# First attention of a two-layer MLP kernel: where the row sums are finished, when the first weights are loaded, and how long O keeps two banks

## The chip, the cores and the metric

One NeuronCore of a Trainium2 chip runs the whole kernel. The time is device time in microseconds (us) of one execution; the median of three executions is compared. One further execution was recorded by the profiler, and all rows below come from it.

## The reference

```python
scores = cap * np.tanh(scale * np.matmul(q, k.transpose(0, 1, 3, 2)) / cap)     # q, k, v: 2 x 12 x 448 x 64
scores = scores - np.max(scores, axis=-1, keepdims=True)
attn = np.exp(scores)
attn = attn / (np.sum(attn, axis=-1, keepdims=True) + 1e-09)
x = np.matmul(attn, v)                                     # then reshaped to 896 tokens x 768
h = x @ w_in                                               # 768 x 2048
x = np.where(h > 0.0, h, np.exp(np.minimum(h, 0.0)) - 1.0) @ w_out
h = x @ w_in2
return np.maximum(0.01 * h, h) @ w_out2
```

## The kernel before

Everything is float32. A product is made of parts: each operand is split into a high part of type float32r and a low part, which is the rest, and hi*hi, hi*lo and lo*hi are added up.

The attention of the 24 heads and most of the first product of the first MLP run in a common loop of 55 steps s (STEPS), which every engine writes out in its own order. A head h has two halves, k = 2h and 2h + 1; a half is 224 rows of the scores. The work of half k is spread over the steps:

- step k - 1: TensorE (PE) makes the scores of half k (`score`, L1080 and L1081), after the tanh of half k - 1 has left the bank.
- step k: ScalarE (ACT) takes the tanh (L598); VectorE (DVE) takes the maximum of each row (`maxima`, L762).
- step k + 1: ACT takes the exponential, two instructions, with the sums of the rows (`exp`, L608).
- step k + 2: PE transposes the probabilities (`transposes`, L1094); ACT copies the high part out (`p_high`, L617); DVE makes the low part (`p_low`, L769).

The work of a whole head stands at these places:

- step 2h + 3: GpSimd (POOL) adds EPS to the row sums (`denominators`, L544), and DVE inverts them (`invert`, L779). The inverse goes to DRAM by a DMA of 1.8 KB at step 2h + 4 (`store_inv`, L443), and comes back spread over 64 rows at step 2h + 5 (`load_inv`, L460). `invert(h)` waits until the store of head h - 2 has landed, since both use one buffer.
- step 2h + 5: PE multiplies by v (`values`): for h < DIRECT = 8 twelve matmuls with 64 rows of output (L1107 to L1109), else eight with 128 rows (L1112, L1113).
- step 2h + 8, for h < 8: DVE multiplies O by the inverse and stores it (`scale_o`, L787). Step 2h + 6, for h >= 8: DVE adds the two halves of O (`take_o`, L797 and L799). Each ends with the semaphore o_read.
- `x_parts(m)` on POOL splits the rows of two heads, 2m and 2m + 1, at step 4m + 11, or 4m + 9 from m = 4 on. `split_v` on POOL splits v, `split_qk` q and k.

All DMAs but one are issued by SyncE (SP) in one order; an issue that waits holds up all behind it. At step 8 it loads four units of the weights (L466), 384 KB each, and at step 29 three more. Three of them are split early: the high part by DVE at steps 11, 15 and 19 (`w_high`, L809), the low part by POOL at steps 13, 17 and 21.

PSUM has eight banks: two for scores, two for the transposed probabilities, two for O (o_ps), two more (mlp_ps) that serve the odd halves below ALONE_P = 22 and then the MLP. `values(h)` may start when enough heads have been read:

```python
        def o_bank(h):
            return o_ps[:, h % 2 if h < DIRECT else 0, 0:SEQ]

        def o_users(h):

            return h - 1 if h <= DIRECT and h >= 2 else h if h > DIRECT else 0
```

From step 24 on the MLP is mixed in. EARLY names unit and chunks for steps 24 to 30, MIXED for the later ones; a chunk is three matmuls (L1118 to L1120). Units 0, 1 and 2 have the banks mlp_ps 0, mlp_ps 1 and o_ps 1. From about step 24 on PE has work in all gaps, and after the attention come the rest of the MLP and the second one.

Of the kernel before, what the change touches and what calls it, by code (L numbers as in the profile page):

```python
# [9 lines left out]
ALU = mybir.AluOpType  # L10
AX = mybir.AxisListType

BATCH, HEADS, SEQ, HD = 2, 12, 448, 64
# [4 lines left out]
NHEAD = BATCH * HEADS  # L18
# [12 lines left out]
RAW = 4  # L31
RING = 4
AHEAD = 3
# [3 lines left out]
EPS = 1e-9  # L37
# [4 lines left out]
ALONE_P = 22  # L42

DIRECT = 8
EARLY = {24: ((2, (0, 1, 2)),), 25: ((2, (3,)),), 26: ((0, (0, 1, 2)),), 27: ((0, (3,)),), 28: ((1, (0, 1, 2)),),
         29: ((1, (3,)),), 30: ((0, (4,)), (1, (4,)), (2, (4,)))}
STEPS = 55
MLP_BANKS = 3

# [14 lines left out]
def chunks_at(s):  # L64

    if s in EARLY:
        return [], [], EARLY[s]
# [94 lines left out]
def build(nc, qT, kT, v, w, cap, out, inv_rows):  # L162
    with ExitStack() as ctx:
# [15 lines left out]
        row_sum, row_den, row_inv = sb("row_sum", [QT, 2, NQ]), sb("row_den", [QT, 2, NQ]), sb("row_inv", [QT, 2, NQ])  # L179
# [67 lines left out]
        o_ps = pb("o_ps", [P, 2, 512])  # L247
# [12 lines left out]
            return slice((h + 1) % 2 * HD, (h + 1) % 2 * HD + HD)  # L260

        def o_bank(h):
            return o_ps[:, h % 2 if h < DIRECT else 0, 0:SEQ]

        def o_users(h):

            return h - 1 if h <= DIRECT and h >= 2 else h if h > DIRECT else 0

        def bank(i):
            return (scores, probs_t, o_ps, mlp_ps)[i // 2][:, i % 2, 0:SEQ]  # L270
# [13 lines left out]
        def unit_hidden(u):  # L284
# [15 lines left out]
        exp_done, transposed, p_hi_done, p_lo_done = (sem("exp_done"), sem("transposed"), sem("p_hi_done"),  # L300
                                                      sem("p_lo_done"))
        den_done, inv_done = sem("den_done"), sem("inv_done")
# [119 lines left out]
        @block.sync  # L422
        def _(sp):
            def load_k(h):
                if h >= 4:
                    sp.wait_ge(k_split, h - 3)
                elif h >= 2:
                    sp.wait_ge(k0_split, h - 1)
                sp.dma_start(k_raw[:, h % 2, :], kT[h, :, :]).then_inc(k_loaded[h % 2], 16)

            def load_q(h):
                if h >= 2:
                    sp.wait_ge(q_split, h - 1)
                sp.dma_start(q_raw[:, h % 2, :], qT[h, :, :]).then_inc(q_loaded[h % 2], 16)

            def load_v(h):
                if h >= 2:
                    sp.wait_ge(v_split, h - 1)
                sp.dma_start(v_raw[:, h % 2, :], v[h, :, :]).then_inc(v_loaded[h % 2], 16)

            def store_inv(h):
                sp.wait_ge(inv_done, h + 1)
                sp.dma_start(inv_rows[h, :].rearrange("(p t) -> p t", t=NQ), row_inv[:, h % 2, :]  # L443
                             ).then_inc(inv_stored[h % 2], 16)

            def load_inv(h):

                m = h // 2
                sp.wait_ge(inv_stored[h % 2], 16 * m + 16)
                if h < DIRECT:  # L450
                    if h >= 2:
                        sp.wait_ge(o_read, h - 1)
                    rows = inv_all[0:HD, h % 2, :]
                else:
                    if m < DIRECT // 2 + 2:
                        sp.wait_ge(o_read, DIRECT - 1 + m - DIRECT // 2)
                    else:
                        sp.wait_ge(x_scaled, m - 1 - DIRECT // 2)
                    rows = inv_all[hi_rows(h), m % 2, :]
                sp.dma_start(rows, inv_rows[h:h + 1, :].broadcast_to([HD, SEQ])  # L460
                             ).then_inc(inv_loaded[h % 4], 16)

            def load_w(r):
                if r >= RAW:
                    sp.wait_ge(*load_free(r - RAW))
                sp.dma_start(w_raw[:, r % RAW, :], w[RAW_ROWS[r], :, :]).then_inc(w_loaded[r % RAW], 16)  # L466

            load_q(0)
            sp.dma_start(cap_col[:, :], cap.broadcast_to([P, 1])).then_inc(cap_loaded, 16)
            load_k(1)  # L470
            load_q(1)
            load_v(0)
            load_v(1)
            for h in (2, 3):
                load_k(h)
                load_q(h)
            for s in range(STEPS):
                for u in units_ending_at(s - 1):
                    load_w(u + AHEAD + RAW)
                if s % 2 == 0 and s // 2 + 4 < NHEAD:  # L480
                    load_k(s // 2 + 4)
                    load_q(s // 2 + 4)
                if s == 8:
                    for u in range(RAW):
                        load_w(u)
                if s % 2 == 1 and 0 <= (s - 5) // 2 < NHEAD:
                    load_inv((s - 5) // 2)
                if s % 2 == 1 and 2 <= s // 2 + 1 < NHEAD:
                    load_v(s // 2 + 1)
                if s % 2 == 0 and 0 <= (s - 4) // 2 < NHEAD:  # L490
                    store_inv((s - 4) // 2)
                if s == 29:
                    for u in range(RAW, AHEAD + RAW):
                        load_w(u)
            for r in range(units_ending_at(STEPS - 1)[0] + AHEAD + RAW, len(RAW_ROWS)):
                load_w(r)
            for i, (there, rows_half, batch) in enumerate(((y12_done, 0, 1), (y22_done, 1, 1), (y11_done, 0, 0), (y21_done, 1, 0))):
                for t in range(HC):
                    sp.wait_ge(there, HC + t + 1)
                    sp.dma_start(out[rows_half * HC + t, :, batch * SEQ:(batch + 1) * SEQ], y_out[:, HC * i + t, :]  # L500
                                 ).then_inc(y_stored, 16)
            sp.wait_ge(y_stored, 16 * BATCH * KC)

        @block.gpsimd
        def _(pool):
# [23 lines left out]
            def split_v(h):  # L529
                b = h % 2  # L530
                pool.wait_ge(v_loaded[b], 16 * (h // 2) + 16)
                if h >= 2:
                    pool.wait_ge(pv_done, h - 1)
                raw = v_raw[:, b, :].rearrange("p (c d) -> p c d", c=NQ)
                pool.tensor_scalar(v_both[:, b, :, hi_rows(h)], raw, 1.0, 0.0, ALU.mult, ALU.add).then_inc(v_hi_done, 1)
                pool.wait_ge(v_hi_done, h + 1)
                pool.tensor_tensor(v_both[:, b, :, lo_rows(h)], raw, v_both[:, b, :, hi_rows(h)].bitcast(F32), ALU.subtract
                                   ).then_inc(v_split, 1)

            def denominators(h):  # L540
                pool.wait_ge(exp_done, 4 * h + 4)
                if h >= 2:
                    pool.wait_ge(inv_done, h - 1)
                pool.tensor_scalar(row_den[:, h % 2, :], row_sum[:, h % 2, :], EPS, 1.0, ALU.add, ALU.mult  # L544
                                   ).then_inc(den_done, 1)

            def x_parts(m):
                b = m % 2
                pool.wait_ge(o_read, 2 * m + 2)
# [23 lines left out]
            for s in range(STEPS):  # L573
                for u in units_ending_at(s - 1):
                    split_w(u + AHEAD)
                if s % 2 == 1 and 0 <= (s - 3) // 2 < NHEAD:
                    denominators((s - 3) // 2)
                for m in range(PAIRS):
                    if s == x_step(m):
                        x_parts(m)  # L580
                if s % 2 == 0 and s // 2 + 2 < NHEAD:
                    split_qk(s // 2 + 2)
                if s % 2 == 1 and 0 <= s // 2 - 1 < NHEAD:
                    split_v(s // 2 - 1)
                if s in (13, 17, 21):
                    split_w((s - 13) // 4)
            for n in LO_ON_POOL[units_ending_at(STEPS - 1)[0] + AHEAD:]:
# [168 lines left out]
        def _(dve):  # L756
# [16 lines left out]
                    ALU.subtract).then_inc(p_lo_done, 1)  # L773

            def invert(h):
                dve.wait_ge(den_done, h + 1)
                if h >= 2:
                    dve.wait_ge(inv_stored[h % 2], 16 * (h // 2))
                nc.vector.reciprocal(row_inv[:, h % 2, :], row_den[:, h % 2, :]).then_inc(inv_done, 1)  # L779
# [282 lines left out]
        def _(pe):  # L1062
# [59 lines left out]
            def hidden(u, chunks):  # L1122
                pe.wait_ge(*split_done(u))
                if u < 2:
                    pe.wait_ge(p_lo_done, ALONE_P)
                elif u == 2:
                    pe.wait_ge(o_read, DIRECT)
                else:
                    pe.wait_ge(g_done, u - MLP_BANKS + 1)
                for c in chunks:  # L1130
                    x = KC * (u // MAT_UNITS) + c
                    if u % MAT_UNITS < MLP_BANKS:
                        pe.wait_ge(x_lo_done, x + 1)
                    last = product(unit_bank(u), u % RING, c, x_hi[:, x, :], x_lo[:, x, :], c == 0, c == KC - 1)
                if KC - 1 in chunks:
                    last.then_inc(unit_done, 1)
# [125 lines left out]
```

## Time and profile before

| what | value |
|---|---|
| three executions | 584.12, 584.13 and 587.40 us; median 584.13 |
| profiled execution | 588.14 us, its span 586.4 us |
| busy share of the span | PE 96%, DVE 79%, ACT 60%, POOL 48% |
| granted TensorE clock, mean | 0.994 of full speed |

The span is the time from the first to the last instruction. Granted clock 1.00 is 2.4 GHz and 0.50 is 1.2 GHz. PE is shown as busy to the modelled end of each matmul, some 0.37 us after its start, while matmuls of 448 columns follow each other at 0.20 us: an idle time that is shown for PE is about 0.2 us shorter than the delay of the next start.

### The profile page before, as it was taken

To read this page: it belongs to the slowest core of one execution; us is meant where nothing else is said; L and a number is where in the kernel's file an instruction comes from. 1 tells how busy PE (TensorE), PEld (TensorE's weight loads), DVE (VectorE), ACT (ScalarE), POOL (GpSimd) and SP (SyncE) were. 2 spreads that over 40 slices of the span, in tenths; PEclk is the share of its full clock that TensorE was granted. 3 is DMA by queue.
4 is the path that set the end of the run, shared out by engine and by line. 5 is a ranking of instruction groups with operands and counts; after the bars stand their busy time and mean duration, and the time that the engine had idled before them with its cause. 6 is when DMAs were issued, how large, how long until landed. Compare 5 with 4: busy or idle time off the path is not lost. (4 is left out here: it accounts for less than half of the span.)

```text
span 586.4 us, 8605 instructions
## 1 busy us (share of the span) xinstructions
PE 560.9 (96%) x2908; PEld 502.9 (86%) x2908; DVE 463.6 (79%) x707; ACT 354.0 (60%) x606; POOL 283.9 (48%) x297
## 2 busy tenths in 40 slices
PE   7898989999999999999999999989999998999997
PEld 5666769888988999999999999969999997899997
DVE  5788888877776323699898989789999868999881
ACT  6998888889997355655554454355445445554440
POOL 6779998898985676554000000687657530000000
PEclk9999989989999999999999999999999999999999
DMA  6364533545433233333743533022111335446241
GB/s 172 89 186 101 137 95 96 174 123 135 116 82 72 78 107 109 108 107 108 269 135 109 182 90 105 1 88 75 54 55 57 96 91 167 156 135 215 82 157 59
DMA packets 34172, 67.07 MB, mean 114 GB/s; under 512 B 6864, under 2 KB 18768, under 8 KB 34128
## 3 DMA queue, kind: packets, MB, share of 16 engines
q1 hardware_dynamic: 33984, 66.28, 38.0%
q8 instruction: 24, 0.39, 0.3%
q10 hardware_dynamic: 144, 0.23, 0.1%
q14 instruction: 20, 0.16, 0.1%
HBM read 63.70 MB, written 2.80 MB: 113 GB/s over the span
## 5 line engine op out<-in xcount | busy, mean ns | idle before, releaser
L564 POOL TENSOR_TENSOR w_lo<-w_raw,w_hi 128x768 fp32r<-128x768 f32 (+1 forms) x62 | 105.5, 1704 | 52.5 <-ACT w_hi L628 51.9
L564 POOL TENSOR_TENSOR w_lo<-s_sum,w_hi 128x384 fp32r<-128x384 f32 x32 | 37.7, 1191 | 119.1 <-ACT w_hi L628 119.1
L628 ACT ACTIVATE w_hi<-s_sum 128x768 fp32r<-128x768 f32 (+1 forms) x64 | 43.4, 684 | 78.4 <-DVE s_sum L880 52.0
L628 ACT ACTIVATE w_hi<-w_raw 128x768 fp32r<-128x768 f32 (+1 forms) x77 | 56.5, 736 | 31.0 <-PE o_ps L1120 15.7
L608 ACT ACTIVATE soft<-soft,neg_max 112x448 f32<-112x448 f32 x96 | 63.0, 661 | 2.7 <-DVE soft L762 2.7
L762 DVE TENSOR_SCALAR_CACHE_REDUCE soft<-soft,neg_abs 112x448 f32<-112x448 f32 x96 | 60.6, 668 | 2.3 <-ACT soft L598 2.0
L769 DVE TENSOR_TENSOR p_lo<-probs_t,p_hi 112x896 fp32r<-112x896 f32 x37 | 40.3, 1089 | 21.9 <-ACT p_hi L617 21.7
L1118 PE MATMUL mlp_ps<-x_hi,w_hi 128*128 128x448 f32 x132 | 49.7, 376 | 0.0
L1120 PE MATMUL mlp_ps<-x_hi,w_lo 128*128 128x448 f32 x132 | 48.7, 369 | 0.0
L1119 PE MATMUL mlp_ps<-x_lo,w_hi 128*128 128x448 f32 x132 | 48.7, 369 | 0.0
L598 ACT ACTIVATE soft<-scores 112x896 f32<-112x896 f32 x47 | 43.0, 914 | 7.4 <-PE scores L1081 7.4
L1080 PE MATMUL scores<-k_hi,q_stack 128*112 128x448 f32 x94 | 37.3, 396 | 6.2 <-ACT soft L598 6.1
L617 ACT ACTIVATE p_hi<-probs_t 112x896 fp32r<-112x896 f32 x37 | 33.7, 910 | 14.1 <-PE probs_t L1094 14.1
L1094 PEld LDWEIGHTS probs_t<-ident,soft 112*112 112x112 f32 x296 | 30.5, 134 | 11.0 <-issue 6.5
L1094 PE MATMUL probs_t<-ident,soft 112*112 112x112 f32 x296 | 34.8, 261 | 5.1 <-DVE p_lo L769 4.0
L1081 PE MATMUL scores<-k_lo,q_stack 128*112 128x448 f32 x94 | 35.1, 373 | 0.0
L804 DVE SCALAR_TENSOR_TENSOR b<-act_g,mlp_ps 128x448 f32<-128x448 f32 x22 | 13.6, 619 | 27.1 <-ACT act_g L637 27.1
L880 DVE TENSOR_TENSOR s_sum<-w_raw 128x768 f32<-128x768 f32 (+1 forms) x32 | 28.7, 896 | 5.9 <-issue 3.6
L884 DVE TENSOR_TENSOR w_lo<-s_sum,w_hi 128x768 fp32r<-128x768 f32 x32 | 30.5, 953 | 1.3 <-ACT w_hi L628 1.3
L839 DVE TENSOR_TENSOR g_first<-b,g_first 128x896 fp32r<-128x896 f32 x24 | 30.1, 1253 | 0.8 <-ACT g_first L647 0.8
L839 DVE TENSOR_TENSOR g_last<-b,g_last 128x896 fp32r<-128x896 f32 x24 | 27.9, 1163 | 2.2 <-ACT g_last L647 2.2
L635 ACT ACTIVATE act_g<-mlp_ps 128x448 f32<-128x448 f32 x22 | 11.9, 540 | 24.9 <-PE mlp_ps L1120 24.9
(236 smaller groups left out, 1753.1 us busy)
## 6 DMA issues: line engine op xcount, KB each, us to landing
w_raw<-w_units SPq DMA_DIRECT2D x120, 384.0 KB, 3.2
q_raw<-qT SPq DMA_DIRECT2D x24, 224.0 KB, 3.0
k_raw<-kT SPq DMA_DIRECT2D x23, 224.0 KB, 2.7
v_raw<-v_rows SPq DMA_DIRECT2D x24, 112.0 KB, 2.8
inv_all<-inv_rows SPq DMA_DIRECT2D x24, 112.0 KB, 3.1
y_t<-y_out SPq DMA_DIRECT2D x12, 224.0 KB, 2.8
inv_rows<-row_inv SPq DMA_DIRECT2D x24, 1.8 KB, 3.0
k_raw<-kT ACTq DMA_DIRECT2D x1, 224.0 KB, 3.3
```

What stands on the lines that cost most here:

```text
L564: pool.tensor_tensor(w_part(w_lo, n), w_source(n), f32(w_part(w_hi, n)), ALU.subtract).then_inc(w_lo_pool, 1)
L598: nc.scalar.activation(soft[0:QT, k % SOFT, :, :], scores_of(k)[0:QT, :, 0:SEQ], ACT.Tanh, scale=scale_reg).then_inc(tanh_done, 1)
L608: nc.scalar.activation(soft[0:QT, b, t, :], soft[0:QT, b, t, :], ACT.Exp, bias=neg_max[:, c, t:t + 1], scale=-1.0, accum_out=row_sum[:, h ...
L628: nc.scalar.activation(w_part(w_hi, n), w_source(n), ACT.Copy).then_inc(w_hi_done, 1)
L762: nc.vector.tensor_scalar(soft[0:QT, b, t, :], soft[0:QT, b, t, :], neg_abs[0:QT, 0:1], BIG, ALU.mult, ALU.min, accum_out=neg_max[:, c, t: ...
L769: nc.vector.tensor_tensor(p_lo[:, h % 2, :, cols].rearrange("p (a b) q -> p a b q", a=2), probs_of(k)[0:QT, :, 0:SEQ].rearrange("p a (b q) ...
L839: nc.vector.tensor_tensor(parts[:, 2:4, :], g_source(l, n)[0], f32(parts[:, 0:2, :]), ALU.subtract).then_inc(g_split, 1)
L1080: nc.tensor.matmul(dst[0:QT, t, 0:SEQ], q_stack[:, b, rows], k_hi[:, b, :], start=True, stop=False)
L1094: last = nc.tensor.transpose(probs_of(k)[0:QT, c // 2, col:col + QT], soft[0:QT, k % SOFT, t, c * QT:(c + 1) * QT], ident[:, :])
L1118: nc.tensor.matmul(dst, w_hi[:, r, blk], hi, start=start, stop=False)
L1119: nc.tensor.matmul(dst, w_hi[:, r, blk], lo, start=False, stop=False)
L1120: return nc.tensor.matmul(dst, w_lo[:, r, blk], hi, start=False, stop=stop)
```

## The change

The EPS is added on DVE, just ahead of the reciprocal, and not on POOL. The seven first units of weights are loaded one by one at steps 7, 11, 15, 19, 23, 26 and 29. O has two banks for ten heads and not for eight; so units 0 and 1 are begun ahead of unit 2. On POOL `split_v` stands ahead of `x_parts`.

```diff
+TWO_BANKS = 10
-EARLY = {24: ((2, (0, 1, 2)),), 25: ((2, (3,)),), 26: ((0, (0, 1, 2)),), 27: ((0, (3,)),), 28: ((1, (0, 1, 2)),),
-         29: ((1, (3,)),), 30: ((0, (4,)), (1, (4,)), (2, (4,)))}
+EARLY = {24: ((0, (0, 1, 2)),), 25: ((0, (3,)),), 26: ((1, (0, 1, 2)),), 27: ((1, (3,)),), 28: ((2, (0, 1, 2)),),
+         29: ((2, (3,)),), 30: ((0, (4,)), (1, (4,)), (2, (4,)))}
+FIRST_LOADS = (7, 11, 15, 19, 23, 26, 29)
...
         def o_bank(h):
-            return o_ps[:, h % 2 if h < DIRECT else 0, 0:SEQ]
+            return o_ps[:, h % 2 if h < TWO_BANKS else 0, 0:SEQ]
         def o_users(h):
-            return h - 1 if h <= DIRECT and h >= 2 else h if h > DIRECT else 0
+            return h - 1 if h <= TWO_BANKS and h >= 2 else h if h > TWO_BANKS else 0
...
-                if s == 8:
-                    for u in range(RAW):
-                        load_w(u)
...
-                if s == 29:
-                    for u in range(RAW, AHEAD + RAW):
-                        load_w(u)
+                if s in FIRST_LOADS:
+                    load_w(FIRST_LOADS.index(s))
...
-            def denominators(h):
-                pool.wait_ge(exp_done, 4 * h + 4)
-                if h >= 2:
-                    pool.wait_ge(inv_done, h - 1)
-                pool.tensor_scalar(row_den[:, h % 2, :], row_sum[:, h % 2, :], EPS, 1.0, ALU.add, ALU.mult
-                                   ).then_inc(den_done, 1)
...
             for s in range(STEPS):
                 for u in units_ending_at(s - 1):
                     split_w(u + AHEAD)
-                if s % 2 == 1 and 0 <= (s - 3) // 2 < NHEAD:
-                    denominators((s - 3) // 2)
+                if s % 2 == 1 and 0 <= s // 2 - 1 < NHEAD:
+                    split_v(s // 2 - 1)
                 for m in range(PAIRS):
                     if s == x_step(m):
                         x_parts(m)
                 if s % 2 == 0 and s // 2 + 2 < NHEAD:
                     split_qk(s // 2 + 2)
-                if s % 2 == 1 and 0 <= s // 2 - 1 < NHEAD:
-                    split_v(s // 2 - 1)
...
             def invert(h):
+                dve.wait_ge(exp_done, 4 * h + 4)
+                nc.vector.tensor_scalar(row_den[:, h % 2, :], row_sum[:, h % 2, :], EPS, 1.0, ALU.add, ALU.mult
+                                        ).then_inc(den_done, 1)
                 dve.wait_ge(den_done, h + 1)
...
                 if u < 2:
                     pe.wait_ge(p_lo_done, ALONE_P)
                 elif u == 2:
-                    pe.wait_ge(o_read, DIRECT)
+                    pe.wait_ge(o_read, TWO_BANKS)
```

The queue of SP at steps 7 to 9, before: the three rows of head 1 (store, load, v), then k and q of head 8, then the weights, then the store of head 2.

```order
L443 DMA inv_rows<-row_inv 112x4
L460 DMA inv_all<-inv_rows 64x448
L439 DMA v_raw<-v_rows 112x256
L429 DMA k_raw<-kT 128x448
L434 DMA q_raw<-qT 128x448
L466 DMA w_raw<-w_units 128x768 x4
L443 DMA inv_rows<-row_inv 112x4
```

The same place in the changed kernel:

```order
L447 DMA inv_rows<-row_inv 112x4
L464 DMA inv_all<-inv_rows 64x448
L443 DMA v_raw<-v_rows 112x256
L470 DMA w_raw<-w_units 128x768
L433 DMA k_raw<-kT 128x448
L438 DMA q_raw<-qT 128x448
L447 DMA inv_rows<-row_inv 112x4
```

One unit in place of four is ahead of the store of head 2, and it stands ahead of k and q; the next ones stand in the same way ahead of the stores of heads 4, 6, 8 and 10.

PE at step 24, with the semaphores that it waits for (the scores of half 25, then the first chunk of the MLP), before:

```order
L1080 MATMUL scores<-k_hi,q_stack 112x448 [waits tanh_done]
L1081 MATMUL scores<-k_lo,q_stack 112x448
L1080 MATMUL scores<-k_hi,q_stack 112x448
L1081 MATMUL scores<-k_lo,q_stack 112x448
L1118 MATMUL o_ps<-x_hi,w_hi 128x448 [waits x_lo_done,o_read,w_lo_pool]
```

and in the changed kernel:

```order
L1074 MATMUL scores<-k_hi,q_stack 112x448 [waits tanh_done]
L1075 MATMUL scores<-k_lo,q_stack 112x448
L1074 MATMUL scores<-k_hi,q_stack 112x448
L1075 MATMUL scores<-k_lo,q_stack 112x448
L1112 MATMUL mlp_ps<-x_hi,w_hi 128x448 [waits x_lo_done,p_lo_done,w_lo_pool]
```

The first chunk now goes to a bank that the odd halves used, and waits for the low part of half 21 where it waited for the reading of O.

## Rows read from the trace of the kernel before

**Rows 1.** The page's granted TensorE clock, 40 slices of 14.7 us.

```profile
PEclk9999989989999999999999999999999999999999
```

**Rows 2.** Stretches of span: PE, PEld, DVE, ACT, POOL busy us; clock, DMA share, GB/s.

```profile
82.30:85.70 3.40, 3.36 (x10) 2.96 (x11) 3.35 (x10) 1.60 (x5) 3.15 (x6) 0.50 0.60 164
89.00:114.00 25.00, 25.00 (x154) 22.96 (x153) 20.82 (x46) 21.08 (x43) 21.93 (x29) 1.00 0.39 108
...
119.90:123.30 3.40, 3.40 (x11) 3.00 (x10) 3.00 (x6) 3.37 (x6) 3.40 (x3) 0.51 0.87 249
```

**Rows 3.** Timeline, steps 10 to 13: start, length, what, idle before and its releaser.

```profile
38.63 1.09 DVE L769 TENSOR_TENSOR p_lo<-probs_t,p_hi 112x896 fp32r<-112x896 f32 x1 [1.05 <-ACT p_hi L617]
...
39.56 0.43 PE L1080 MATMUL scores<-k_hi,q_stack 128*112 128x448 f32 x1 [0.33 <-ACT soft L598]
...
39.75 0.96 DVE L787 TENSOR_TENSOR x_raw<-o_ps,inv_all 64x448 f32<-64x448 f32 x1
...
40.86 0.39 PE L1107 MATMUL o_ps<-p_hi,v_both 112*64 112x448 f32 x1 [0.27 <-DVE x_raw L787]
...
44.28 0.92 ACT L617 ACTIVATE p_hi<-probs_t 112x896 fp32r<-112x896 f32 x1 [0.66 <-PE probs_t L1094]
...
45.09 0.92 ACT L598 ACTIVATE soft<-scores 112x896 f32<-112x896 f32 x1
```

**Rows 4.** Timeline of PE: first score matmul of steps 9, 13, 15 and 17.

```profile
33.06 0.43 PE L1080 MATMUL scores<-k_hi,q_stack 128*112 128x448 f32 x1 [0.33 <-ACT soft L598]
...
46.16 0.43 PE L1080 MATMUL scores<-k_hi,q_stack 128*112 128x448 f32 x1 [0.33 <-ACT soft L598]
...
53.16 0.43 PE L1080 MATMUL scores<-k_hi,q_stack 128*112 128x448 f32 x1 [0.33 <-ACT soft L598]
...
60.82 0.43 PE L1080 MATMUL scores<-k_hi,q_stack 128*112 128x448 f32 x1 [0.33 <-ACT soft L598]
```

**Rows 5.** Waits of PE, 0 to 190 us: in total, times, longest.

```profile
PE probs_t L1094 <- DVE p_lo L769: 4.0, 4, 1.8
PE o_ps L1107 <- DVE x_raw L787: 2.7, 5, 1.3
```

**Rows 6.** Timeline of SP's queue, steps 6 to 11.

```profile
29.73 0.43 SPq L443 DMA_DIRECT2D inv_rows<-row_inv  x1
32.12 0.45 SPq L460 DMA_DIRECT2D inv_all<-inv_rows  x1
...
35.88 1.86 SPq L466 DMA_DIRECT2D w_raw<-w_units  x4
37.77 0.60 SPq L443 DMA_DIRECT2D inv_rows<-row_inv  x1
43.65 0.45 SPq L460 DMA_DIRECT2D inv_all<-inv_rows  x1
```

**Rows 7.** Timeline of DVE, steps 11 to 14: what waited for a DMA.

```profile
43.73 0.18 DVE L779 RECIPROCAL row_inv<-row_den 112x4 f32<-112x4 f32 x1 [0.69 <-DMA inv_rows<-row_inv]
...
51.03 0.18 DVE L779 RECIPROCAL row_inv<-row_den 112x4 f32<-112x4 f32 x1 [1.11 <-DMA inv_rows<-row_inv]
...
54.43 0.95 DVE L787 TENSOR_TENSOR x_raw<-o_ps,inv_all 64x448 f32<-64x448 f32 x1 [1.04 <-DMA inv_all<-inv_rows]
```

**Rows 8.** Timeline of DVE, PE and ACT, steps 22 to 25.

```profile
78.80 1.09 DVE L769 TENSOR_TENSOR p_lo<-probs_t,p_hi 112x896 fp32r<-112x896 f32 x1 [0.35 <-ACT p_hi L617]
...
79.93 0.96 DVE L787 TENSOR_TENSOR x_raw<-o_ps,inv_all 64x448 f32<-64x448 f32 x1
...
82.34 0.71 PE L1112 MATMUL o_ps<-p_hi,v_both 112*128 112x448 f32 x1 [1.58 <-DVE x_raw L799]
...
83.42 0.67 ACT L608 ACTIVATE soft<-soft,neg_max 112x448 f32<-112x448 f32 x1 [0.94 <-DVE soft L762]
...
88.99 0.93 PE L1094 MATMUL probs_t<-ident,soft 112*112 112x112 f32 x8
```

**Rows 9.** Groups by line, 0 to 190 us: busy us, mean ns, idle before.

```profile
L544 POOL TENSOR_SCALAR row_den<-row_sum 112x4 f32<-112x4 f32 x24 | 4.6, 193 | 2.0
```

## The prediction

> **What bounds the kernel now.** I read the page's clock row first, then the stretches, then the chain of starts in the attention. From 89 to 114 us PE has no idle time at full clock [rows 2]; up to step 24, about 85 us, it waits now and then. So time can only be won ahead of 89 us, and a wait that ends there moves all that follows.
>
> Ahead of step 24 the loop over a head closes like this, read off steps 10 to 13 [rows 3]. The scores start at 39.56, just behind a tanh; `values` of head 3 starts at 40.86, where it would follow the four score matmuls at 40.4 (four at 0.2 and the longer first one). It waits for `scale_o`, which ends at 40.71, and this stands in DVE's order behind `p_low`, which waited 1.05 us for ACT. Everything after `values` is late with it: the transposes, the high part at 44.28 (0.66 us late by ACT's account), and behind it, in ACT's order, the tanh at 45.09, which lets the next scores start. So the distance between two score starts is the price of a head, waits included. With the one at 39.56 [rows 3], the starts 33.06, 46.16, 53.16 and 60.82 [rows 4] give 6.50 (head 2), 6.60 (head 3), 7.00 (head 4) and 7.66 us (head 5). The waits behind them are 2.7 us in five times, the longest 1.3 [rows 5].
>
> Heads 2 and 3 run with no DMA in the way, so 6.50 for an even head and 6.60 for an odd one is what this order costs. Heads 4 and 5 are longer by 0.50 and 1.06. There DVE waited for DMAs: 0.69 and 1.11 us in `invert`, 1.04 in `scale_o` [rows 7]. And there the queue of SP shows why: the store at 29.73 had landed 2.4 us later, when the load that waits for it was issued at 32.12; the store at 37.77, behind four units of weights, landed after 5.9 us, at 43.65 [rows 6]. SP waits at that place, so v, k, q and the next store are late too, which is how head 5 pays.
>
> The second place is step 23. `values(9)` starts at 82.34 after 1.58 us of idle PE, released by the second half of `take_o(8)` [rows 8]: heads 8 and 9 share a bank. The clock is at 0.50 from 82.3 to 85.7, that is 1.2 GHz, and PE is busy for 3.36 of these 3.40 us [rows 2], so this stretch costs 1.7 us. It began when PE took up work after that wait. A like stretch, 119.9 to 123.3, costs 1.7 more [rows 2]; its wait, 1.8 us for `p_low`, is the longest of four [rows 5]. The clock row has these two dips and no other [rows 1].
>
> That bears on the base of the sum. The three times are 584.12, 584.13 and 587.40: the third is 3.3 above the others, about two such stretches (3.4). The profiled execution, 588.14, has both; without them it would be 584.7. I take it that the median, 584.13, has neither.
>
> **The change part by part.**
>
> *Loads one by one.* At step 7 one unit stands ahead of the store of head 2 in place of four. The four made the landing 5.9 instead of 2.4 us, 3.5 for four, so 0.9 us for one: a landing of about 3.3 us. SP reaches that store 1.9 us earlier too, since the one unit now stands ahead of k and q [rows 6]. So it lands at about 35.9 + 3.3 = 39.2. `invert(4)`, which needs it, could start about 43.0 (43.73 less its wait of 0.69 [rows 7]): 3.8 us to spare. The three DMA waits of DVE go, and heads 4 and 5 fall back to 6.50 and 6.60. Gain 0.50 + 1.06 = **1.56 us**, bounds 1.0 (part of head 5's time is POOL's or ACT's) and 2.2 (head 3's wait shrinks also). At step 29 one unit in place of three; PE waits for nothing there (89 to 114 us [rows 2]), so it is worth 0. The units that are split early are wanted at steps 11, 15 and 19, four steps of over 3 us after their load: nothing waits.
>
> *EPS on DVE.* It takes 0.19 us on POOL, 24 times, 4.6 us in all [rows 9]. On DVE the nearest row is the reciprocal of the same tile, 0.18 us [rows 7]. If all of it were seen, it would cost 24 x 0.19 = 4.6 us. But it stands ahead of `maxima` at odd steps, and DVE waits for ACT after that, ahead of `p_low`: 1.05 us at step 10 [rows 3], 0.35 at step 22 [rows 8], where it is tightest. 0.18 fits into 0.35, so I take 0. At step 11 the early `w_high` stands there as well and the margin is nearly used up; 0.1 may show there. The waits of `invert` for POOL go, but DVE waits for ACT next anyway: worth 0 where PE is full.
>
> *Two banks for ten heads.* `values(9)` now waits for `scale_o(7)`, 79.93 + 0.96 [rows 8], so it starts at 81.0, not 82.34: 1.34 us earlier. What is late next? The next point at which PE waits for a vector engine is the transposes of half 23, at 88.99 [rows 8]; 1.7 us of the way there is half clock, so with full clock it stands at 87.3. By PE alone it would now be 86.0. But it needs the low part of half 22: the exponential of half 23 starts at 83.42, held by DVE's `maxima` behind `take_o(8)` (0.94 us [rows 8]), which the bank does not change. Two exponentials and their read-outs take 1.4 us, the high part 0.92, the low part 1.09 [rows 3], the semaphores 0.1: 86.95. So the gain at full clock is 87.3 - 86.95 = **0.35 us**, bounds 0 (EPS on DVE pushes that low part back by 0.18, and more) and 1.34 (if `maxima` gets earlier by itself). In an execution like the profiled one it is 88.99 - 86.95 = 2.05, since the half clock would go with the wait. The first chunk of the MLP, which now waits for the low part of half 21, comes at about 84.3, when DVE has just finished it (it precedes the reciprocal of step 23): at most 0.2 us, inside the margin of the same chain. `values(10)` needs `take_o(8)` only, and `values(11)` as before.
>
> *v first on POOL.* POOL shows no wait that PE pays for in this part; `values` is released by O alone [rows 5]. `x_parts` moves back by about 1.2 us of v and gains 0.3 of the EPS; its rows are first used at step 24, the nearest pair five steps after its split. Worth 0.
>
> Sum: 1.56 + 0.35 = 1.9 us. From the median 584.13 this gives **582.2 us**. For a profiled execution: 588.14 - 1.56 - 2.05 = 584.5 if the second stretch at half clock stays, and 582.8 if both are missing.
>
> **A rule that speaks against the spread loads.** The small store landed after 5.9 us behind four units [rows 6]. The Trainium skill, "DMA: Bandwidth & Descriptors", section "Queues, rings and completion order", says that a completion increment lands only after every earlier write of the same DMA engine; by that rule, the trace agrees, any unit ahead of a store is paid by the store, and now five stores have one ahead of them instead of one store four.
>
> **The rivals.**
>
> *Slower: five stores late instead of one.* Each load ahead of a store delays its landing, and `invert` two heads later waits for it on DVE. If each of the five cost what the worse of the two heads costs, 1.06 us, it would be 5.3 us for a gain of 0.35 at the bank: 584.13 + 5.3 - 1.56 - 0.35 = 587.5. Against it: with a landing of 3.3 us there are 3.8 us to spare. It decides once a store takes longer than about 7.1 us to land.
>
> *Nothing to see.* DVE fills the gaps: with EPS on it and `w_high` at three steps, heads 4 and 5 stay late by other waits, and the chain of step 23 eats the bank's gain. Then 583.7 to 584.4.
>
> *The clock.* The wait of 1.8 us at step 33 remains, and whether a half clock follows a wait differs between executions. If the median now has one stretch, 582.2 + 1.7 = 583.9, with both 585.6. The other way round, if the median of before had the first stretch and this one has not, the gain is 1.56 + 2.05 = 3.6, and 580.5.
>
> *The full price of DVE.* If EPS is seen in all the heads ahead of step 24, ten of them, 1.8 us: 584.0.
>
> **How the numbers follow.** Forecast, 581.3 to 583.2: 0.50. Nothing to see or EPS seen, 583.2 to 584.4: 0.20. One stretch at half clock more, 583.9 to 585.6: 0.10. Late stores, 585 to 588: 0.07. Gain of 3 us or more, 579.5 to 581.3: 0.10. Something else: 0.03. The range 580.2 to 585.2 leaves out about 0.15. A change of this kernel can be told from none from about 1% on, 5.8 us. Faster by that would need three times the sum above, which no term here gives: 0.03; slower: 0.03; within 1%: 0.94.
>
> **What the profile after would show.** SP: the store of head 2 lands within 3.5 us. DVE: no wait of `invert` or `scale_o` for a DMA up to step 20, and none for row_den. Score starts of steps 13 to 17 at distances of 6.5 and 6.6. `values(9)` within 0.6 us of its scores' end, and the transposes of half 23 released by `p_low`, some 3 us after the exponential of half 23 has started. The clock at 1.00 in step 23. The prediction is wrong if stores take over 6 us again, if `p_low` no longer waits for ACT at even steps (then DVE is the bound), or if the steps behind 33 are not the same length as before.

## The result, and the profile after

| what | before | after |
|---|---|---|
| median of 20 runs | 585.70 us (583.90 to 588.87) | 589.23 us (586.79 to 595.62) |
| profiled execution | 588.14 us, span 586.4 | 593.0 us, span 591.1 |
| mean granted clock there | 0.994 | 0.994 |

The ratio is 1.0053, 95% interval 1.0036 to 1.0069: slower by 3.1 us, where 1.9 us faster was forecast. The execution of 595.62 us counts as a slow one and is left out of the ratio. The result is within the 1% given 0.94, and the median is above the range (585.2). The lines of the changed kernel stand some 6 to 10 lines earlier in its code: L1080 is now L1074, L779 is L773, L787 is L781. The EPS is added in L768.

The page's clock row, which answers to [rows 1], and two of the stretches of [rows 2] (columns as there):

```profile
PEclk9999988999999999999999999999999999999999
```

```profile
85.30:92.20 6.90, 6.59 (x22) 5.86 (x23) 5.82 (x15) 3.82 (x8) 1.84 (x3) 0.51 0.31 94
92.20:114.00 21.80, 21.80 (x134) 19.95 (x133) 19.73 (x43) 18.08 (x37) 18.82 (x24) 1.00 0.40 104
```

There is one dip where there were two, but it is 6.9 us long, 3.4 us lost, as much as both of before together. So the half clock makes none of the 4.9 us between the two profiled executions. PE has no idle time from 92 to 114 us, as it had none from 89 to 114 before [rows 2], so what changed lies ahead of 92 us here too.

The timeline of PE, first score matmul of steps 9, 11, 13, 15, 17, 19 and 21, which answers to [rows 4]:

```profile
32.99 0.43 PE L1074 MATMUL scores<-k_hi,q_stack 128*112 128x448 f32 x1 [0.33 <-ACT soft L589]
39.49 0.43 PE L1074 MATMUL scores<-k_hi,q_stack 128*112 128x448 f32 x1 [0.33 <-ACT soft L589]
46.10 0.43 PE L1074 MATMUL scores<-k_hi,q_stack 128*112 128x448 f32 x1 [0.33 <-ACT soft L589]
52.59 0.43 PE L1074 MATMUL scores<-k_hi,q_stack 128*112 128x448 f32 x1 [0.33 <-ACT soft L589]
60.32 0.43 PE L1074 MATMUL scores<-k_hi,q_stack 128*112 128x448 f32 x1 [0.33 <-ACT soft L589]
67.14 0.43 PE L1074 MATMUL scores<-k_hi,q_stack 128*112 128x448 f32 x1 [0.33 <-ACT soft L589]
74.53 0.43 PE L1074 MATMUL scores<-k_hi,q_stack 128*112 128x448 f32 x1 [0.33 <-ACT soft L589]
```

Head 4 (46.10 to 52.59) costs 6.49 us, the forecast 6.50. Head 5 costs 7.73, head 6 6.82 and head 7 7.39, though the queue of SP has lost its hold-up. Its timeline at steps 8 and 9, answering to [rows 6]:

```profile
35.78 0.43 SPq L447 DMA_DIRECT2D inv_rows<-row_inv  x1
38.87 0.45 SPq L464 DMA_DIRECT2D inv_all<-inv_rows  x1
```

The store of head 2 is in after 3.1 us, where it took 5.9. None of the stores up to step 24 takes more than 3.7 us, and DVE waits for no DMA there. So something else holds heads 5 to 7. The waits of PE, 0 to 190 us (in total, times, longest), answer to [rows 5]:

```profile
PE o_ps L1106 <- DVE x_raw L781: 4.5, 2, 3.9
...
PE o_ps L1101 <- DVE x_raw L781: 3.2, 4, 1.4
PE probs_t L1088 <- DVE p_lo L760: 2.8, 3, 1.8
```

`values` waits for DVE's `scale_o`, once for 3.9 us. Why DVE is late shows its timeline at step 21 (start, length, what):

```profile
77.11 1.07 DVE L760 TENSOR_TENSOR p_lo<-mlp_ps,p_hi 112x896 fp32r<-112x896 f32 x1
78.12 3.99 DVE L768 TENSOR_SCALAR row_den<-row_sum 112x4 f32<-112x4 f32 x1
82.14 0.18 DVE L773 RECIPROCAL row_inv<-row_den 112x4 f32<-112x4 f32 x1
82.23 0.65 DVE L753 TENSOR_SCALAR_CACHE_REDUCE soft<-soft,neg_abs 112x448 f32<-112x448 f32 x1
```

The addition of EPS to 112x4 numbers took 3.99 us. The timeline of POOL beside it:

```profile
77.38 0.74 POOL L537 TENSOR_TENSOR v_both<-v_raw,v_both 112x256 fp32r<-112x256 f32 x1
78.07 1.84 POOL L557 TENSOR_TENSOR w_lo<-w_raw,w_hi 128x768 fp32r<-128x768 f32 x1
79.87 0.57 POOL L511 TENSOR_SCALAR k_hi<-k_raw 128x448 fp32r<-128x448 f32 x1
80.41 0.57 POOL L520 TENSOR_SCALAR q_stack<-q_raw 128x448 fp32r<-128x448 f32 x1
80.94 1.14 POOL L523 TENSOR_TENSOR k_lo<-k_raw,k_hi 128x448 fp32r<-128x448 f32 x1
82.04 1.12 POOL L526 TENSOR_TENSOR q_stack<-q_raw,q_stack 64x448 fp32r<-64x448 f32 x1
```

`row_den` begins 0.05 us after POOL's `w_lo` and ends at 82.11, 0.03 us after the end of `k_lo`: four instructions of POOL without a gap lie over it. What stands behind it on DVE is `maxima` of half 22, `p_low` of half 20, and `scale_o(7)`; from all engines' timeline, who waits for them (the exponential of half 22, then `values(9)`):

```profile
83.53 0.67 ACT L599 ACTIVATE soft<-soft,neg_max 112x448 f32<-112x448 f32 x1 [3.01 <-DVE soft L753]
...
84.52 0.94 DVE L781 TENSOR_TENSOR x_raw<-o_ps,inv_all 64x448 f32<-64x448 f32 x1
...
85.61 0.71 PE L1106 MATMUL o_ps<-p_hi,v_both 112*128 112x448 f32 x1 [3.90 <-DVE x_raw L781]
```

This is the place of [rows 8]. There `values(9)` waited 1.58 us for `take_o(8)`. Now it needs `scale_o(7)` only, as the banks were meant to bring about, and waits 3.90 for that. The half clock begins at 85.3, at the end of that wait.

The groups by line, whole span (busy us, mean ns, idle before), for L768:

```profile
L768 DVE TENSOR_SCALAR row_den<-row_sum 112x4 f32<-112x4 f32 x24 | 19.4, 810 | 0.0
```

19.4 us in 24 times, where POOL took 193 ns each [rows 9] and I had taken 0.18. Its shortest took 0.15 us, its median 0.51. Of the 19.4 us, 10.9 lie ahead of 92 us; behind that PE has no idle time up to 114 us.

The prediction had named a sign of being wrong: that `p_low` no longer waits for ACT at even steps, since then DVE is the bound. It came true. Before, `p_low` waited 1.05 us for ACT at step 18 and 0.35 at step 22; in the changed kernel it waits for ACT at no step from 12 to 23.

### The profile page after: what moved, and what is told of

Same layout as the page of the kernel before. It is cut to its first block and busy times, and to the rows that moved or that the text cites. A ratio compares the mean times of both kernels' runs of the same rounds, so it can differ in the third digit from the quotient of the medians.

```text
span 591.1 us, 8583 instructions
## 1 busy us (share of the span) xinstructions
PE 562.8 (95%) x2908; PEld 502.0 (85%) x2908; DVE 482.5 (82%) x731; ACT 354.6 (60%) x606; POOL 277.8 (47%) x273
## 5 line engine op out<-in xcount | busy, mean ns | idle before, releaser
L1074 PE MATMUL scores<-k_hi,q_stack 128*112 128x448 f32 x94 | 37.5, 399 | 6.4 <-ACT soft L589 5.0
L1106 PE MATMUL o_ps<-p_hi,v_both 112*128 112x448 f32 x64 | 24.4, 382 | 4.5 <-DVE x_raw L781 4.5
```

Of the source, the lines that this page charges most:

```text
L1074: nc.tensor.matmul(dst[0:QT, t, 0:SEQ], q_stack[:, b, rows], k_hi[:, b, :], start=True, stop=False)
```

## The experiments

Four kernels each were run on one chip, together with the kernel before, whose median stands below them. Microseconds are worked out from the ratios; a difference between two ratios is good to about 1.4 us, going by their intervals.

| run | median us | ratio to before, 95% |
|---|---|---|
| EPS back on POOL | 584.16 | 0.9969 (0.9952 to 0.9987) |
| EPS on DVE alone | 590.20 | 1.0068 (1.0043 to 1.0093) |
| EPS on DVE in another form | 583.99 | 0.9962 (0.9945 to 0.9978) |
| loads alone | 585.94 | 0.9987 (0.9966 to 1.0008) |
| (before, beside these four) | 586.47 | |
| w_lo a step later | 585.71 | 0.9980 (0.9963 to 0.9997) |
| loads and banks | 585.15 | 0.9971 (0.9954 to 0.9988) |
| banks alone | 584.89 | 0.9976 (0.9960 to 0.9991) |
| other form, take_o later | 584.16 | 0.9961 (0.9939 to 0.9983) |
| (before, beside these four) | 586.89 | |

### EPS back on POOL (eps_back_on_pool)

The changed kernel with this one part undone.

```diff
+            def denominators(h):
+                pool.wait_ge(exp_done, 4 * h + 4)
...
+                pool.tensor_scalar(row_den[:, h % 2, :], row_sum[:, h % 2, :], EPS, 1.0, ALU.add, ALU.mult
+                                   ).then_inc(den_done, 1)
...
             def invert(h):
-                dve.wait_ge(exp_done, 4 * h + 4)
-                nc.vector.tensor_scalar(row_den[:, h % 2, :], row_sum[:, h % 2, :], EPS, 1.0, ALU.add, ALU.mult
-                                        ).then_inc(den_done, 1)
```

> The changed kernel with the EPS back on POOL, in its old place; loads, banks and v first stay. Theory A (the EPS instruction on DVE is held up by instructions of POOL that run beside it, up to 3.99 us in step 21 of the changed kernel): without it on DVE the three other parts give what was forecast, 1.9 us faster than before, 1.0 to 2.5, and no DVE instruction of 4 columns lasts over 0.3 us. Theory B (DVE is simply full, any instruction more in its queue is late): the same result here. Theory C (v first pushes POOL's other work back, and that holds DVE up): still 2 to 4 us slower than before.

Measured 0.9969, that is 1.8 us faster than before; against the changed kernel's 1.0053 it is 0.0084, or 4.9 us. So EPS on DVE costs about 5 us, and theory C (v first) is out. The other three parts together give what the sum had for them (1.9), by luck: the runs of single parts below put one term lower than the sum had it and one higher. In its profiled execution the clock is 1.00 throughout, and step 23 is as forecast, in PE's timeline: `values(9)` early (though 0.85 us behind its scores, where 0.6 was given), the transposes of half 23 released by the low part.

```profile
79.66 0.44 PE L1112 MATMUL o_ps<-p_hi,v_both 112*128 112x448 f32 x1 [0.85 <-DVE x_raw L787]
...
85.54 0.95 PE L1094 MATMUL probs_t<-ident,soft 112*112 112x112 f32 x8 [0.33 <-DVE p_lo L769]
```

### EPS on DVE alone (eps_on_dve_alone)

The kernel before with this part only: `denominators` goes from POOL, and `invert` has the three lines that are taken out above.

> The kernel before with the EPS on DVE and nothing else changed. Theory A: row_den has a mean over 0.4 us on DVE with single ones over 1.5 us, and the kernel is slower than before by 2 to 6 us, about the 4.7 us by which step 25 came later in the changed kernel plus the 1.9 us that the other parts would give. Theory B: slower as well, but every row_den lasts under 0.25 us. Theory C: within 0.5 us of before.

1.0068, 4.0 us slower than before. Its groups by line give 801 ns for one. At step 21, from the timeline, with POOL's instructions around it:

```profile
77.37 0.74 POOL L537 TENSOR_TENSOR v_both<-v_raw,v_both 112x256 fp32r<-112x256 f32 x1
...
77.78 2.21 DVE L768 TENSOR_SCALAR row_den<-row_sum 112x4 f32<-112x4 f32 x1
...
78.06 1.85 POOL L557 TENSOR_TENSOR w_lo<-w_raw,w_hi 128x768 fp32r<-128x768 f32 x1
...
79.86 0.58 POOL L511 TENSOR_SCALAR k_hi<-k_raw 128x448 fp32r<-128x448 f32 x1
...
84.81 0.44 PE L1106 MATMUL o_ps<-p_hi,v_both 112*128 112x448 f32 x1 [3.42 <-DVE x_raw L793]
```

It ends at 79.99, 0.08 us after `w_lo`, and the wait of `values(9)` is 3.42 where it was 1.58. The loss is in this part, with no help from the others, and theory B, every `row_den` under 0.25 us, is out.

### The same addition on DVE, in another form (eps_dve_accum_form)

The one that tells DVE's load from the wait beside POOL: the addition keeps its place and engine, and has an output of its accumulator as well (the minimum with 3e38 changes no value), which adds an instruction that reads it out.

```diff
-                nc.vector.tensor_scalar(row_den[:, h % 2, :], row_sum[:, h % 2, :], EPS, 1.0, ALU.add, ALU.mult
-                                        ).then_inc(den_done, 1)
+                nc.vector.tensor_scalar(row_den[:, h % 2, :], row_sum[:, h % 2, :], EPS, BIG, ALU.add, ALU.min,
+                                        accum_out=den_min[:, :]).then_inc(den_done, 1)
```

> The changed kernel with the EPS on DVE in the form that L753 uses, which also writes an accumulator output (add EPS, then the smaller of that and 3e38: the values are the same). DVE's queue is as full as in the changed kernel, and a read-out of 0.08 us is added. Theory A, in its narrower form (only the plain form is held up by POOL): no row_den over 0.4 us, and the time is that of the run with the EPS on POOL within 0.7 us, so 1 to 2 us faster than before. Theory B: as slow as the changed kernel or slower, 3 us over before. Theory C: the same, 3 us over before.

0.9962: the loss is gone, 5.3 us by the ratios (1.0053 less 0.9962). The groups by line:

```profile
L768 DVE TENSOR_SCALAR_CACHE_REDUCE row_den<-row_sum 112x4 f32<-112x4 f32 x24 | 3.5, 144 | 0.0
...
L768 DVE DVE_READ_ACCUMULATOR row_den<-row_sum 112x1 f32 x24 | 1.9, 81 | 0.0
```

The longest of the 24 took 0.155 us, though POOL works beside them as before. So it is neither the place in DVE's order nor the work of 0.2 us, but the plain form waiting for POOL. With 0.23 us per head on DVE the time is that of EPS on POOL (0.9969) within the intervals: the step "0.18 fits into 0.35" holds for this form. `p_low` still waits for ACT at step 22, 0.20 us.

### w_lo a step later (w_lo_a_step_later)

POOL's 1.84 us low part of a first unit goes behind `split_qk`, one step later, so that it does not lie over `invert` at steps 13, 17 and 21.

```diff
-                if s in (13, 17, 21):
-                    split_w((s - 13) // 4)
+                if s in (14, 18, 22):
+                    split_w((s - 14) // 4)
```

> The changed kernel with one edit: POOL's three early splits of weights (1.84 us each, right behind v at steps 13, 17 and 21) stand one step later, behind the splits of k and q. DVE's own queue is word for word that of the changed kernel. Theory A (a plain EPS instruction waits until POOL, working without a gap, lets it in): the three worst cases, 2.24, 1.92 and 3.99 us, all of which begin just ahead of such a split, fall to under 0.9 us; the wait of 3.90 us of PE at step 23 goes; the kernel is within 1.5 us of the run with the accumulator form, about 584.5 to 585.5. Rival (a plain instruction with a short row on DVE is slow at random or by its own queue, and POOL's neighbours do not matter): as the changed kernel, 2.5 to 3.5 us slower than before.

0.9980, so 4.3 us of the loss went by the ratios, with EPS still on DVE in its plain form. The three worst, 2.24, 1.92 and 3.99 us, became 0.45, 0.50 and 0.49; others grew (1.54 at 89.98), and the mean is 596 ns. DVE's timeline at step 21, then PE's at step 23 and at the transposes:

```profile
75.98 0.49 DVE L768 TENSOR_SCALAR row_den<-row_sum 112x4 f32<-112x4 f32 x1
```

```profile
79.98 0.45 PE L1106 MATMUL o_ps<-p_hi,v_both 112*128 112x448 f32 x1 [0.41 <-DVE x_raw L781]
...
86.46 0.95 PE L1088 MATMUL probs_t<-ident,soft 112*112 112x112 f32 x8 [0.95 <-DVE p_lo L760]
```

So the lengths follow POOL's neighbours, and the rival, slow at random, is out. What is left of the loss, about 1 us against the accumulator form, is within the intervals of the two, but the last row shows it: the transposes come at 86.46 and not at 85.05.

### Loads alone (loads_alone), banks alone (banks_alone), both (loads_and_banks)

Each is the kernel before with that part of the diff and nothing else; the last lacks of the changed kernel EPS on DVE and v first.

```diff
-                if s == 8:
-                    for u in range(RAW):
-                        load_w(u)
...
+                if s in FIRST_LOADS:
+                    load_w(FIRST_LOADS.index(s))
```

> The kernel before with the seven first weight loads one by one and nothing else. Theory of the prediction: the store of head 2 lands within 3.5 us, the score starts of steps 13, 15 and 17 are 6.5 and 6.6 us apart, PE still waits 1.6 us for the second half of take_o at step 23, and the kernel is 1.0 to 2.2 us faster, 1.56 at the likeliest. Rival (each load ahead of a store makes that store late): five stores land after 5 us or more, DVE waits for DMAs as often or more, 0 to 4 us slower.

0.9987, 0.8 us faster by the ratio, and the interval takes in no change, as well as 1.56. The queue of SP:

```profile
35.92 0.43 SPq L444 DMA_DIRECT2D inv_rows<-row_inv  x1
39.09 0.45 SPq L461 DMA_DIRECT2D inv_all<-inv_rows  x1
```

The store lands within 3.2 us, as worked out, and no store up to step 24 takes over 3.3, so the rival (late stores) is out. But head 4 stays at 6.87 us, and only head 5 falls, to 6.60.

```diff
+TWO_BANKS = 10
...
         def o_bank(h):
-            return o_ps[:, h % 2 if h < DIRECT else 0, 0:SEQ]
+            return o_ps[:, h % 2 if h < TWO_BANKS else 0, 0:SEQ]
```

> The kernel before with the two banks for ten heads and nothing else. By the prediction 0.35 us faster than before where the clock stays full, 2.05 us where the wait was followed by half clock; in the profile PE's wait at step 23 is under 0.9 us, and heads 4 and 5 stay at 7.0 and 7.7 us. Rival (the bank is worth more in the typical execution since half clock follows the long wait often): 1 to 2 us faster.

0.9976, 1.4 us, as the rival had it (1 to 2), and more than the 0.35 of the sum. PE's timeline at step 23 and at the transposes of half 23:

```profile
80.01 0.44 PE L1113 MATMUL o_ps<-p_hi,v_both 112*128 112x448 f32 x1 [0.51 <-DVE x_raw L788]
...
85.89 0.95 PE L1095 MATMUL probs_t<-ident,soft 112*112 112x112 f32 x8 [0.33 <-DVE p_lo L770]
```

The store behind the four units takes 5.7 us to land here, as before, yet head 4 costs 6.90 us and head 5 6.60. Half clock has become rare: 2 of the 12 executions have a mean granted clock of 0.997 or less (one stretch of 3.4 us takes 0.003), against 11 of 12 with the loads alone and 50 of the 64 of the kernel before beside the experiments.

> The kernel before with the loads one by one and the two banks for ten heads; EPS on POOL and v behind x_parts as before. If v first is worth nothing, as the prediction had it: the time of the run with the EPS back on POOL, 1.8 us faster than before, within 0.5 us. If v first is what brings head 4 back to 6.50 us (6.87 us with the loads alone, 6.49 in the run with the EPS back on POOL): 0.3 to 0.5 us slower than that run. PE's wait at step 23 falls from 1.8 us to under 0.9 us, released by the multiplication of O, no longer by take_o.

0.9971. With v first it is 0.9969, so v first is worth nothing that can be told in the time. The sum of loads and banks alone would be 0.9963; the two are about additive within their intervals. The traces show that v first does two things that cancel. Its timeline has

```profile
42.44 1.15 POOL L557 TENSOR_TENSOR x_lo<-x_raw,x_hi 128x448 fp32r<-128x448 f32 x1
...
42.53 1.48 DVE L807 CAST w_hi<-w_raw 128x768 fp32r<-128x768 f32 x1
...
79.59 0.44 PE L1110 MATMUL o_ps<-p_hi,v_both 112*128 112x448 f32 x1 [0.50 <-DVE x_raw L785]
```

The cast of the early weights, 0.53 us elsewhere, lies over POOL's `x_lo` and ends 0.42 us behind it, and head 4 costs 6.87 us. In all six kernels or repeats with v behind `x_parts` head 4 costs 6.83 to 7.47 us; in all six with v first it costs 6.48 to 6.50 (the cast takes 0.95 us in eps_back_on_pool). But there `values(9)` waits 0.85 us and not 0.50: `invert` at step 21 waits for POOL's EPS, and starts at nearly the same time in both, 76.18 and 76.11 us.

### take_o later (accum_take_o_later)

The accumulator form, and `take_o(8)` behind `p_low` of step 23, so that `maxima` of half 23 isn't behind it.

```diff
+                if s == 2 * DIRECT + 7:
+                    take_o(DIRECT)
...
-                if s % 2 == 0 and DIRECT <= (s - 6) // 2 < NHEAD:
+                if s % 2 == 0 and DIRECT < (s - 6) // 2 < NHEAD:
```

> The run with the accumulator form, and take_o of head 8 moved from step 22 to step 23, behind p_low: its bank is wanted again only at step 25. What held the exponential of half 23 was DVE's maxima behind take_o. If the chain from there to the transposes of half 23 is what limits the gain of the banks: their wait for p_low, 0.45 us, gets shorter or goes, and the kernel is 0.2 to 0.5 us faster than that run, 583.5 us. Rival (p_low of half 22 is now behind take_o instead): no change, or 0.3 us slower.

0.9961 against 0.9962: nothing, as the rival had it. The transposes of half 23 start at 85.04, against 85.05, after a wait of 0.82 for the low part in place of 0.45. PE came there sooner and waited longer for the same thing.

### Both kernels once more (before_again, after_again)

> The kernel before, once more, for a second profile. What it tells: whether the loss of 0.50 and 1.06 us at heads 4 and 5, on which the prediction's larger term rests, is there in every execution. If it is the rule: score starts of steps 13 to 17 again 7.0 and 7.7 us apart, the second store behind the weights lands after 5 us again. If it belonged to that one execution, as the run with the banks alone suggests (6.90 and 6.60 us with the same four loads in a row): about 6.9 and 6.6.

> The changed kernel, once more, for a second profile. Theory A (the EPS instruction on DVE waits for POOL): again 15 us or more of row_den in all, the longest ones at the steps at which POOL works without a gap (13, 17 and 21), though not the same lengths to the hundredth. Rival (one bad execution): row_den near 0.2 us all along.

Before: 588.62 us in its profiled execution. Two of the score starts of [rows 4] again, steps 15 and 17:

```profile
53.49 0.43 PE L1080 MATMUL scores<-k_hi,q_stack 128*112 128x448 f32 x1 [0.33 <-ACT soft L598]
60.09 0.43 PE L1080 MATMUL scores<-k_hi,q_stack 128*112 128x448 f32 x1 [0.33 <-ACT soft L598]
```

Head 5 costs 6.60 us here, not 7.66; head 4 (from 46.02) costs 7.47, not 7.00. The store of head 2, behind the four units, lands after 5.8 us again; that of head 3 lands after 4.3, where it took 5.2 in the first profile and 2.7 in banks_alone. So the hold-up of the first store is the rule, and what it costs heads 4 and 5 is not: 1.56 us, 0.97, and 0.40 in banks_alone.

After: 590.01 us, `row_den` 17.2 us in all, and at step 21 the timeline has

```profile
77.86 1.83 POOL L557 TENSOR_TENSOR w_lo<-w_raw,w_hi 128x768 fp32r<-128x768 f32 x1
...
78.12 1.59 DVE L768 TENSOR_SCALAR row_den<-row_sum 112x4 f32<-112x4 f32 x1
...
79.74 0.57 POOL L511 TENSOR_SCALAR k_hi<-k_raw 128x448 fp32r<-128x448 f32 x1
```

The same instructions, and this time DVE gets in behind `w_lo` after 1.59 us and not behind `k_lo` after 3.99.

## Why the prediction was wrong

**EPS on DVE: the step that failed.** "0.18 fits into 0.35, so I take 0." The cost that the runs show is 4.0 us with this part alone, and 4.9 and 5.3 us by what the changed kernel gains when EPS goes back to POOL or takes the other form. The duration was taken from the reciprocal of the same tile, which is not held beside POOL: 177 to 179 ns in all 24. The plain TENSOR_SCALAR is. In the four traces that have it on DVE (after, after_again, eps_on_dve_alone, w_lo_a_step_later) 68 of the 96 take over 0.25 us, and every one of these 68 ends within 0.08 us of the end of a POOL instruction; the others, 0.15 to 0.23 us, lie where POOL is idle (15) or where one of its instructions begins or ends within 0.2 us of their start (13). The upper bound, 4.6 us, was made of POOL's duration, so it bounded the work and not the wait: the 24 took 19.4 us, 10.9 of them ahead of 92 us. The loss is less than that; I take the rest to be what DVE's waits for ACT covered, which no run separates.

The Trainium skill, "SBUF — State Buffer", section "Who interferes with whom", says that VectorE and GpSimd share a pair of SBUF ports, that copy, cast and `tensor_scalar` "(not the form that also writes out its accumulator)" can claim it, and that the one that comes second "fully blocks" until the other's instruction is over. The trace agrees, by the 68 ends and by the form with an accumulator. I had not weighed it against this change, and it speaks against it. The 3.99 us over four instructions go beyond "the whole instruction" of the page; there the measurement decides.

The trace of before had a hint as well. Its timeline at step 11:

```profile
42.96 1.15 POOL L559 TENSOR_TENSOR x_lo<-x_raw,x_hi 128x448 fp32r<-128x448 f32 x1
...
43.82 0.70 DVE L809 CAST w_hi<-w_raw 128x768 fp32r<-128x768 f32 x1
...
44.07 0.71 POOL L535 TENSOR_SCALAR v_both<-v_raw 112x256 fp32r<-112x256 f32 x1
```

The cast takes 0.53 us at steps 15 and 19, but 0.70 here beside POOL, and POOL's instruction takes 0.71 in place of 0.41. In loads_alone the same cast started earlier, beside the same `x_lo`, and took 1.47 us; it ended 4.96 us after the score start of step 11 in both, which fits with head 4 staying at 6.87 there.

**The rivals.** "The full price of DVE" had the right engine and the wrong size: 1.8 us at the most, from 0.18 per head. "Slower: five stores late" did not happen; the five landed within 3.7 us, where it wanted 7.1. "Nothing to see" had DVE's gaps used up, with no price for the wait. "The clock" has a share at most: the 3.90 us wait of PE was followed by 6.9 us at 1.2 GHz, but six of the 20 executions of the changed kernel had a mean granted clock of 1.00, and they took 586.8 to 588.4 us, each above the median of before.

**Loads one by one.** The landings came out as worked out, the gain did not: 1.56 us forecast, 0.8 measured, not told from 0 nor from 1.56. The 1.06 us of head 5 was one execution's, since 6.60 us came out in before_again and in banks_alone, with the four loads in a row. And of the 0.50 of head 4, 0.37 stayed with no DMA in the way: it goes with v first, which the prediction put at 0.

**Two banks.** Right in each step: `values(9)` early, the low part of half 22 next. 1.4 us measured, between the 0.35 at full clock and the 2.05 in executions where a half clock goes with the wait. The 0.35 that I put in the sum supposed that the typical execution of before has no such stretch, and by their mean clock 50 of 64 have one or more. That the two terms, 0.8 in place of 1.56 and 1.4 in place of 0.35, add up to about the forecast 1.9 again is luck (the interval of each alone is about 1 us either way).

**The base.** The median of three was 584.13; that of 20 is 585.70, and those beside the experiments were 586.47 and 586.89. The three may well have had a median with neither stretch, but most executions of before have one, so as a base it was too low by about 1.6 us. That alone would have put the forecast at 583.8, inside the range; it does not explain 589.2.

**v first.** 0 in the time, as said, but by two effects of under 0.4 us that cancel and not for want of any. **Behind step 33** nothing changed, as said: from the scores of half 34 to those of half 47 PE took 59.42 us before and 59.49 in after_again; the 58.15 in the profile of the changed kernel lacks the second stretch at half clock.

**Left open.** Behind which of POOL's instructions DVE gets in. In 58 of the 68 cases it is the one that was running. In ten DVE passed over a change: seven times from `v_both` to `w_lo`, twice to the first instruction of `x_parts`, and once (after) from `w_lo` to `k_hi` and over two changes more, while in the same place it got in behind `w_lo` in after_again and in eps_on_dve_alone. No run tells why.

The best kernels here, the accumulator form with or without the later `take_o`, are 2.2 to 2.3 us faster than before by their ratios; whether they beat EPS on POOL (0.9969) lies within the intervals.

## What to carry to other kernels

When a small plain tensor_scalar or cast is moved to VectorE, put beside it what GpSimd runs at that time: its price is up to the rest of GpSimd's instruction, or of a train of them, and not its own duration. Look in the trace for the same kind of instruction taking longer at some places than at others before taking a duration from a neighbour of another kind. Where the operation must be there, a form with an accumulator output, or keeping GpSimd's long instructions out of that step, brought the whole or most of the loss back here. And a base for a forecast wants more than three executions when the kernel has stretches at half clock in some of them.

## What the runs showed of the hardware

- A VectorE tensor_scalar of 112x4 took 0.15 us alone and up to 3.99 us beside GpSimd; the same addition with an accumulator output took 0.13 to 0.155 us in all 24 places, plus 0.08 for the read-out.
- Its wait can pass over the change from one GpSimd instruction to the next, in one case three such changes, and differs between executions of the same program (3.99 and 1.59 us at one place).
- It works both ways: GpSimd's tensor_scalar of 112x256 took 0.71 us beside a VectorE cast, and 0.41 without; the cast took 1.48 us beside GpSimd's `x_lo` (loads_and_banks), and 0.53 without.
- After PE had been idle for 3.90 us, the granted clock was 0.51 for 6.9 us. It did not grow with the wait otherwise: after 1.51 (after_again), 1.58 (before), 1.81 (loads_alone) and 3.42 us idle (eps_on_dve_alone) it was 0.50 for 3.4 us each.
